# A three-stage kernel (attention, routed experts, dense layer): the experts' input rows arrive by quarters and VectorE turns them in 32x32 blocks instead of TensorE

## The reference, cut to what matters

```python
attn_out = softmax(q @ mean_pool(k, 8).T / 8) @ mean_pool(v, 8)   # 4 x 8 heads, 576 tokens, 64 wide
x = attn_out as [2304, 512]                                       # tokens x features
logits = x @ w_gate + log1p(exp(x @ w_noise)) * noise             # 8 experts
two best experts per token, weights softmaxed over the two
for e in range(8):                                                # tokens that chose e
    out += weight * (relu(x @ w1[e]) @ w2[e])                     # 512 -> 1024 -> 512
h = out @ w_in                                                    # 512 -> 2048
result = maximum(0.01 * h, h) @ w_out                             # 2048 -> 512, f32
```

## Time and profile before

| | |
|---|---|
| median of three executions | 1072.41 us (1072.01 to 1073.37) |
| profiled execution, its own time | 1069.9 us |
| its span | 1068.2 us |
| mean granted TensorE clock | 0.989 |
| TensorE busy | 1033.9 us (97%), 5222 instructions |
| TensorE weight loads | 871.3 us (82%) |
| VectorE busy | 360.8 us (34%) |
| ScalarE busy | 272.3 us (25%) |
| GpSimd busy | 398.7 us (37%) |
| DMA, mean | 99 GB/s |

### The profile page before, as it was taken

How to read it: one execution, slowest core, us unless ns; L and a number is a source line. 1 busy time by engine, 2 the same in 40 slices (tenths; PEclk the granted TensorE clock), 3 DMA queues, 4 the chain that set the end, 5 groups by cost and what they waited for, 6 DMA issues and landing times.

```text
span 1068.2 us, 16369 instructions
## 1 busy us (share of the span) xinstructions
PE 1033.9 (97%) x5222; PEld 871.3 (82%) x5223; DVE 360.8 (34%) x652; ACT 272.3 (25%) x498; POOL 398.7 (37%) x453
## 2 busy tenths in 40 slices
PE   5998889999999999999999999999999999999998
PEld 4988668888888888888888887888888888888886
DVE  5886624222222222221212224643323333333222
ACT  3542122222222222222222221322222222222222
POOL 6588880643719073462908208811101000000000
PEclk9997999999999999999999999999999999999999
DMA  8955561342515143351514315411101101001001
GB/s 307 341 179 195 190 202 43 118 119 87 157 49 176 59 137 109 94 151 56 171 59 147 98 39 168 119 41 40 37 4 62 38 20 60 21 1 40 1 1 40
DMA packets 53927, 106.06 MB, mean 99 GB/s; under 512 B 7424, under 2 KB 7552, under 8 KB 53888
## 3 DMA queue, kind: packets, MB, share of 16 engines
q1 hardware_dynamic: 35456, 63.59, 19.2%
q10 hardware_dynamic: 12672, 23.07, 6.7%
q0 software_dynamic: 5760, 18.88, 5.4%
HBM read 77.47 MB, written 28.05 MB: 99 GB/s over the span
## 4 chain that ended last, share of the span: by engine, by line
PE 88%; POOL 5%; DVE 2%; issue 2%; DMA 1%; ACT 0%; SPq 0%; ACTq 0%; POOLq 0%; DVEq 0%
PE ps L730 26%; PE ps L732 26%; PE ps L731 26%; PE ps L756 3%; POOL x_sorted L516 3%; PE ps L737 2%; PE ps L659 2%; PE ps L683 1%; POOL w_split L549 1%; PE ps L844 1%; POOL w_split L547 1%; PE ps L669 1%; DMA k_raw<-in_kT_dram 0%; POOL w_split L493 0%; DVE maxima L1108 0%
## 5 line engine op out<-in xcount | busy, mean ns | idle before, releaser
L549 POOL TENSOR_TENSOR w_split<-w_raw,w_split 128x512 fp32r<-128x512 f32 x144 | 186.2, 1293 | 12.0
L547 POOL TENSOR_SCALAR w_split<-w_raw 128x512 fp32r<-128x512 f32 x144 | 91.4, 635 | 217.4 <-PE ps L732 216.9
L730 PE MATMUL ps<-w_split,hT_hi 128*128 (+1 forms) x344 | 139.2, 405 | 1.2 <-DVE hT_lo L1280 1.2
L730 PE MATMUL ps<-w_split,xs_hi 128*128 (+1 forms) x344 | 137.6, 400 | 2.3 <-issue 2.3
L732 PE MATMUL ps<-w_split,hT_lo 128*128 (+1 forms) x344 | 135.1, 393 | 0.0
L731 PE MATMUL ps<-w_split,hT_hi 128*128 (+1 forms) x344 | 134.5, 391 | 0.0
L732 PE MATMUL ps<-w_split,xs_lo 128*128 (+1 forms) x344 | 134.2, 390 | 0.0
L731 PE MATMUL ps<-w_split,xs_hi 128*128 (+1 forms) x344 | 134.1, 390 | 0.0
L606 POOL DMA_INDIRECT y_in<-y_blocks,y_rows x36 | 34.9, 969 | 254.1 <-DVE x L1411 201.1
L730 PE MATMUL ps<-x_hi,w_split 128*128 128x512 f32 (+1 forms) x320 | 119.4, 373 | 0.6 <-DVE x_lo L1444 0.6
L732 PE MATMUL ps<-x_hi,w_split 128*128 128x512 f32 (+1 forms) x320 | 117.8, 368 | 0.0
(11 more groups left out here) (176 smaller groups left out, 1514.5 us busy)
## 6 DMA issues: line engine op xcount, KB each, us to landing
w_raw<-in_wall_dram SPq DMA_DIRECT2D x160, 256.0 KB
xs<-x_sorted ACTq DMA_DIRECT2D x45, 256.0 KB
y_blocks<-y_sb ACTq DMA_DIRECT2D x43, 256.0 KB, 2.0
k_raw<-in_kT_dram SPq DMA_DIRECT2D x16, 288.0 KB, 5.1
q_sb<-in_qT_dram SPq DMA_DIRECT2D x18, 256.0 KB, 4.5
v_raw<-in_vT_dram SPq DMA_DIRECT2D x16, 288.0 KB, 5.9
out_dram<-h_sb SPq DMA_DIRECT2D x10, 256.0 KB, 2.0
x_sorted<-zero_rows SPq DMA_DIRECT2D x9, 256.0 KB, 4.2
```

Of the source, the lines that this page charges most:

```text
L547: pool.tensor_scalar(hi, w_raw[:, a, :], 1.0, 0.0, ALU.mult, ALU.add).then_inc(split_hi, 1)
L549: pool.tensor_tensor(lo, w_raw[:, a, :], hi.bitcast(F32), ALU.subtract).then_inc(split, 1)
L730: pe.matmul(out_ap, lhs_hi, rhs_hi, start=first, stop=False)
```

## The change

The load of a block's rows becomes four DMAs of 64 KB. DMA a brings the features 128a to 128a+127 of all 128 rows to the partitions 32a to 32a+31: partition 32a+i holds that quarter of the rows i, 32+i, 64+i and 96+i, in four pieces of 512 B. One VectorE instruction then transposes each 32x32 block of `xs` and writes to `XT_BANK`, so that partition 32a+i of column group k holds feature 128a+32k+i for the 128 rows in order. The rows of `w1` are reordered on the host to the same order of features, so the sum over features is the same. TensorE's `turn_rows` with its four transposes is gone; the h values are still transposed by TensorE. VectorE's new instruction stands right ahead of each split_rows.

```diff
+QUAD = 32
+QUADS = P // QUAD
 (TensorE)
-            def turn_rows(b):
-                pe.wait_ge(xs_in, b * 16 + 16)
-                for k in range(KD):
-                    mm = pe.transpose(ps[:, XT_BANK, k * P:(k + 1) * P], xs[:, k * P:(k + 1) * P], ident[:, :])
-                mm.then_inc(xs_turned, 1)
                 for k in range(KF):              # down
-                    if first and k == KF // 2:
-                        turn_rows(b + 1)
-            turn_rows(0)
             up(0, 0)
             up(1, expert_of(1))
-            turn_rows(2)
             turn_h(1)
             with pe.Fori(LISTED_BY, BLOCKS) as b:     # and the blocks 2 to 4 ahead of it
                 up(b, expert_of(b))
-                turn_rows(b + 1)
                 down(b - 1, expert_of(b - 1), False)
                 turn_h(b)
 (ScalarE)
+            def load_by_quads(row):
+                for a in range(QUADS):
+                    act.dma_start(xs[a * QUAD:(a + 1) * QUAD, :].rearrange("i (t c) -> i t c", t=QUADS),
+                                  x_sorted[bass.ds(row, P), a * P:(a + 1) * P].rearrange("(t i) c -> i t c", t=QUADS)
+                                  ).then_inc(xs_in, 16)
             def load_rows(b):                    # load_early alike
-                act.dma_start(xs[:, :], x_sorted[bass.ds(row, P), :]).then_inc(xs_in, 16)
+                load_by_quads(row)
 (VectorE)
+            def turn_rows(b, first=False):
+                dve.wait_ge(xs_in, b * (16 * QUADS) + 16 * QUADS)
+                if not first:
+                    dve.wait_ge(xs_split, b)
+                dve.transpose(ps[:, XT_BANK, :].rearrange("p (k t i) -> p t k i", k=KD, t=QUADS),
+                              xs[:, :].rearrange("p (t k i) -> p t k i", t=QUADS, k=KD)).then_inc(xs_turned, 1)
+            turn_rows(0, True)
             split_rows(0)
             split_h(0)
+            turn_rows(1)
             split_rows(1)
             copy_y(0, True)
+            turn_rows(2)
             split_rows(2)
             split_h(1)
             list_y_rows()
+            turn_rows(3)
             split_rows(3)
             with dve.Fori(4, BLOCKS - 1) as b:
+                turn_rows(b + 1)
                 split_rows(b + 1)
                 copy_y(b - 1, False)
                 split_h(b)
+            turn_rows(BLOCKS)
             split_rows(BLOCKS)
 (host)
-    w1 = inputs['moe_w1'].reshape(EXPERTS, KD, P, F).transpose(0, 2, 1, 3).reshape(EXPERTS, P, KD * F)
+    w1 = inputs['moe_w1'].reshape(EXPERTS, QUADS, KD, QUAD, F).transpose(0, 1, 3, 2, 4).reshape(EXPERTS, P, KD * F)
```

More of the change, by code:

```diff
@@ L1392, in _ @@
             finish_y_rows()
+            turn_rows(4)
             split_rows(4)
```

## The result

The change makes the kernel faster: median 1053.19 us (1052.78 to 1053.42, four executions) against 1072.80 (1072.01 to 1073.37), a ratio of 0.982 with a 95% interval of 0.980 to 0.983. That is 19.6 us off; 18.2 were forecast, and the time lies in the forecast range of 1051.2 to 1057.2. Taken together, 14 executions of the kernel after range from 1048.3 to 1059.2 with a median of 1052.94, and the median of before lay, from one batch of runs to another, between 1070.8 and 1072.8. So differences of 1 or 2 us in what follows are read from traces, not from times.

A forecast was written before the change was run, and what follows sets the result against it. TensorE, 97% busy, was taken to bound the rounds from block 3 on, and scatters the start; 17.8 us from 40 rounds plus 0.4 from the first blocks, 18.2 off 1072.41, gave 1054.2 us, range 1051.2 to 1057.2.

The forecast's parts named there:

- The saving per round: Block loop: four transposes off TensorE save 0.44 us a round, 17.8 us over 40 rounds, ends 17.4 and 20.4.
- the direct difference of two starts: Around TensorE's transposes, from up(b)'s last matmul to down(b-1)'s second: 0.90 - 2 x 0.23 = 0.44 us a round.
- The upper end of 0.51: Everything in a round neither matmul nor turn of h: 12.28 - 48 x 0.227 - 0.87 = 0.51 us, the most saved.
- VectorE's transpose: One VectorE instruction per block: 0.69 us, ends 0.575 and 2.8, free in the loop.
- The cover of 8.1 us: VectorE in the loop: a transpose from 406.42 ending by 414.5 delays nothing, since up(b+1) starts later.
- The quarters: Four DMAs per block: 1.14 us more issue, landing 3.13 + 1.14 = 4.3 us (ends 3.13 and 12.5), free in the loop.
- Rival D: Slower: `xs`'s single-buffer ring decides once landing exceeds 10.5 us; about 1147 us at 12.5 us landing; chance 0.04.
- The first blocks: Blocks 0 to 3: up(0) 1.2 us later, up(2) about 1, absorbed by TensorE's idle time; down(1) earlier, gain 0.4 us.
- rival A: Clock does not fall before down(1), as TensorE's idle time shrinks to some 3.5 us or less: 1052.3 us; chance 0.07.
- B: Start gives some back: VectorE holds up GpSimd's scatters, quarters land slower, or boundary costs more; 1055.5 to 1058.5 us; chance 0.12.
- the boundary without transposes: TensorE, from up(b) to down(b-1): a step of 0.23 us; in rival B, say 0.1 more per round, 4 us.
- C: No change: some other per-round wait of 0.44 us takes the transposes' place; chance 0.02.

The follow-up runs named there:

- ten transposes: Kernel after with VectorE's transpose made ten times per round in 38 rounds, each waiting for the one before: 1097.04 us, 26.1 over before.
- the three experiments that share its first blocks: Kernel after with four or eight unused TensorE transposes added per round, or VectorE's transpose made ten times: 1072.19, 1090.09 and 1097.04 us.
- both moves: Kernel after with ScalarE's copy of h of block 1 ahead of block 3's load and VectorE's block 0 transpose ahead of the last placing: 1048.31, 1047.60 us.

## Why the prediction came out right

**The saving per round** was the right mechanism, and its size was a little low: 0.44 forecast, 0.49 measured, over 40 rounds 19.7 in place of 17.8 us. The term that was mis-sized is the direct difference of two starts around the transposes, which left out that the nine matmuls behind them start 0.232 us apart and not 0.227. The upper end of 0.51, worked out from the length of the whole round, had this in it.

**VectorE's transpose** cost 0.72 for 0.69 forecast, and was free as argued. The cover of 8.1 us was wrong, however: ten transposes showed about 6.8, and 5.6 in rounds with slow loads. The step that failed followed the transposed rows to up(b+1) and named what is queued behind the transpose on VectorE, but not that ScalarE's copy of h waits behind xs_hi and the issues in ScalarE's list. With a single transpose it makes no difference.

**The quarters** were free in the rounds. Issue took 1.85 us for four where 4 x 0.34 with gaps of 0.04 gives 1.5, and a quarter landed 2.1 us after its issue in the median. By the median the last one is there about 1.5 + 2.1 = 3.6 us after the first issue. In block 1, where it counted, VectorE could start 4.9, 4.1 and 4.7 us after it in the three traces, around the 4.3 of the sum. Rival D had asked for 10.5.

**The first blocks** went wrong in their parts, and that their total is near the forecast is luck. From the last scatter to up(3), the kernel after takes 14.7 to 14.9 us in three traces (14.92, 14.69, 14.66) and 14.5 to 14.9 in the three experiments that share its first blocks (14.88, 14.55, and 14.94 with ten transposes), before 15.4 in two: 0.4 to 0.9 us gained for 0.4 forecast. But down(1) did not start 0.73 us earlier than before. Counted from the last scatter's issue it started 0.8 us later in the first trace (8.55 for 7.76), since up(2) ended late and the four issues ahead of the store and the copy took 2.9 us and not 1.5. It won that back because it ran at full clock, 5.6 us for 24 matmuls where before needed 6.8. That is rival A's event, and its condition held more strongly than rival A had said: TensorE idled 1.29, 1.56 and 0 us in front of down(1) in the three traces, since it was late by itself.

The forecast had it 1.2 us late at up(0), which is right (up(0) stands 2.17 us behind the end of placing, where it was 0.93), and about 1 us at up(2). It missed that the wait of 3.2 us before up(0) would cost clock there (7.2, 8.0 and 7.8 us for the 24 matmuls in three traces, where before took 5.6 in two), and that block 1 would have to wait for its quarters. From up(0) to up(2) the kernel after took 27.1, 25.3 and 27.3 us, before 23.2 and 22.8. In the first trace up(2) so started 4.3 us later than before, counted from the last scatter. Of these, 2.6 went into the idle time in front of down(1), which shrank from 3.88 to 1.29, 0.9 into the transposes of block 3 that no longer stand there, and 0.8 is what down(1) was late.

**The other rivals.** B's collision of VectorE with GpSimd doesn't occur: GpSimd's low split took 1.29 us beside the transpose, and its means over 144 are 633 and 1294 ns against 635 and 1293. The Trainium skill, page "SBUF — State Buffer", section "SBUF: two separate sides", has VectorE hold the ports that it shares with GpSimd when it has two SBUF inputs or runs in a two-port mode, and VectorE's transpose with its one SBUF input agrees with that. The other part of B, the boundary without transposes, measured 0.23 us as taken. C and D did not occur. The Trainium skill, page "DMA: Bandwidth & Descriptors", section "Anatomy of one DMA — SWDGE (gpsimd) path", says of DMAs that GpSimd issues that most of a small one's time is fixed. On ScalarE's queue the trace goes the same way: 2.1 us for 64 KB, where 256 KB were 3.13 us.

**What stays open.** The part behind up(3) became 19.5 to 19.8 us shorter, by the traces, and the medians of single batches differ by 19.6, 18.0 and 18.7. So what stands ahead of up(3) gained nothing at the end and may have lost up to 1.8 us, where the sum has a gain of 0.4; the executions scatter too much to say which. It isn't S3, and no delay of the last scatter shows either: it is issued at 141.3 to 146.1 us in the eight traces whose work up to it is that of the kernel after (mean 144.1), and at 142.5, 144.2 and 145.4 in the three that begin like before (mean 144.0). Rival B's "the start gives some back" is therefore neither shown nor ruled out, at a size of about a microsecond.

## What to carry to other kernels

Where one engine has no gap over hundreds of microseconds, an instruction taken off its list is worth its start-to-start cost plus what the switch of kind does to its neighbours. The whole round divided by its repeats shows both, and one difference of starts doesn't. The cover of work that is moved to another engine is its round less everything that follows it there in order, waits for third engines included. Such a cover is measured by repeating the work until the round grows. And in the start of a pipeline the order of a few instructions decides: the transpose one step earlier and one copy ahead of a load gave about a quarter of the change's own gain again (4.5 against 18.7 us in one batch).

## What the runs showed of the hardware

VectorE transposes 128x512 f32 in 32x32 blocks from SBUF into PSUM in 0.72 us, where its subtraction of that size takes 0.69. Four TensorE transposes of 128x128 f32, added behind four others, cost 0.43 us, and the switch back to matmuls about 0.07 us once. A DMA issue of ScalarE takes 0.33 us, four in a row 1.8 to 2.0 as a rule; single ones took up to 1.16, 1.07 and 1.02 us in the three traces of after. Quarters of 64 KB landed 2.1 us after their issue in the median and 5.3 at most. TensorE's waits of 3.2 us before up(0) were followed by matmuls at 0.43 us, the level of 1.2 GHz, in two traces at the first matmul and in one at the sixth, with the same wait. With both moves it waited 1.75 us there in one trace and kept the full clock, and 1.82 us in the other and began at 1.2 GHz; before, 1.48 us were followed by the full clock in both traces. Where the low level falls in a kernel with short waits varies from execution to execution.
